# Attention's chunk loads wait for the landing of the load two chunks ahead, the first weights' load for the one ahead of it

## The chip, the cores and the metric

The kernel runs on one NeuronCore of a Trainium2 chip. The metric is the device time of one execution in microseconds (us); lower is better. TensorE (PE) multiplies matrices, VectorE (DVE), ScalarE (ACT) and GpSimd (POOL) work on elements, SyncE (SP) issues most of the DMAs, ScalarE's queue a few.

## The reference

Three layers, each on the output of the one before, all in fp32:

```python
def _attn_ref(q, k, v):            # batch 4, 8 heads, 768 steps, head_dim 64
    for t in range(S):
        state = gamma * state + einsum('bhd,bhe->bhde', k[:, :, t], v[:, :, t])
        y[:, :, t] = scale * einsum('bhd,bhde->bhe', q[:, :, t], state)

def _moe_ref(x, w_in, w_out):      # 3072 tokens, 512 -> 2048 -> 512
    h = maximum(x @ w_in, 0.0)
    return h * h @ w_out

def _moe2_ref(x, w_gate, w_val, w_out, rms_g):   # 512 -> 1536 -> 512
    xn = x / sqrt(mean(x * x) + 1e-6) * rms_g
    g = xn @ w_gate
    return silu(g) * (xn @ w_val) @ w_out
```

## The kernel before, in words

**Attention** is done in chunks of 128 steps, 24 of them (4 batches by 6 chunks, `NCH = 24`, `CH = 6`). A chunk's q, k, v and k by token lie side by side in DRAM, 1024 KB in all; a batch's last chunk needs no k by token and loads 768 KB. The chunks go into a ring of five places in SBUF, `qkv_sb[:, n % RING]` with `RING = 5`. For chunk n TensorE multiplies k by q into scores (L794), VectorE masks them (L1340); TensorE then multiplies q by the running state (L813), updates the state (L845) and multiplies v by the masked scores (L822), whose last product counts `chunk_done`. The scores of chunk n+1 are made before the rest of chunk n, so TensorE needs the load of n+1 when it begins its turn n. ScalarE scales k two chunks ahead (L973) and stores the outputs of 16 of the 24 chunks to DRAM on its own DMA queue, 256 KB each (L961); the outputs of the other eight stay in SBUF. VectorE copies the outputs out of PSUM (L1329).

**The two expert layers** follow in three tiles of 1024 tokens each. Every product is made by Strassen's scheme of seven products, and every one of these by three fp32r products of a high and a low part (L871 to L873). For this ScalarE rounds an operand to its high part and GpSimd or VectorE subtracts that from it to get the low part. A group of weights ("m") is four blocks in `raw_w`, 1024 KB; its sums and parts go to `w_ops`. The weights of the second matrices are prepared once, as 49 "items" of 512 KB that are stored to DRAM (L476) and later loaded back. The first 14 items are prepared during attention, from two sets of raw weights loaded into `raw_w` in four halves of 512 KB (L464), and some wait in places of `ops` that the first expert products need: those products start with attention's end, and ScalarE may write their operands only when the items are stored.

**The order of the loads** is written by hand in SyncE's program (L478 to L505), one queue, in this order: tables and the first three chunks in halves (L443, L446), chunks 3 and 4 (`load_chunk`, L451), then for each n from 0 to 18: wait until chunk n is done and its place is free, load chunk n+5; behind chunk 6 the first weights (`load_raw_w(0)`, L458), behind chunks 9, 11, 16 and 17 one half of the items' raw weights, behind chunk 13 the gains (2 KB). Then come the stores of the 14 items, the first two ahead of the second weights (L503), twelve behind. A load's landing is told by a semaphore of its place: `chunk_ready(n)` (L424) names the semaphore and the count for chunk n, and TensorE, ScalarE and GpSimd wait for it. GpSimd (`first_sums`, `low_w`) and ScalarE (`high_w`) work on the first weights from chunk 4 on.

Of the kernel before, what the change touches and what calls it, by code (L numbers as in the profile page):

```python
# [40 lines left out]
RING = 5  # L41
# [75 lines left out]
def updates_by(n):  # L117
    b, c = divmod(n, CH)
    return (CH - 1) * b + min(c + 1, CH - 1)
# [18 lines left out]
def build(nc, qkv, decay_rows, tables, w_f1, w_f2, w_b, rms_g, out):  # L138
# [6 lines left out]
    with ExitStack() as ctx:  # L145
# [278 lines left out]
        def chunk_ready(n):  # L424

            return loaded[n % RING], 16 * (n // RING + 1)
# [14 lines left out]
        def _(sp):  # L441
# [3 lines left out]
            def load_first_kv(n):  # L445
                sp.dma_start(qkv_sb[:, n, V:K + 1], qkv[0, n, :, V:K + 1, :]).then_inc(loaded[n], 16)  # L446

            def load_chunk(n):
                b, c = divmod(n, CH)
                kinds = 4 if c < CH - 1 else 3  # L450
                sp.dma_start(qkv_sb[:, n % RING].rearrange("p a d -> p (a d)")[:, 0:kinds * DM],  # L451
                             qkv[b, c].rearrange("p a d -> p (a d)")[:, 0:kinds * DM])\
                    .then_inc(loaded[n % RING], 16)

            def load_raw_w(m):
                src = w_f1[m % R1] if m < M1 else w_f2[(m - M1) % R2]
                dst = raw_w[:, m % 2].rearrange("p a k d -> p (a k d)")
                sp.dma_start(dst, src).then_inc(raw_w_loaded[m % 2], 16)  # L458

            def load_early_quad(quad, half):  # L460

                src = w_b[quad].rearrange("p (a d) -> p a d", a=4)[:, 2 * half:2 * half + 2, :]
                dst = raw_w[:, 1 - quad, 2 * half:2 * half + 2].rearrange("p a k d -> p a (k d)")
                sp.dma_start(dst, src).then_inc(quad_loaded[0], 16)  # L464
# [17 lines left out]
            load_first_kv(1)  # L482
            load_first_kv(2)
            for n in range(FIRST, RING):
                load_chunk(n)
            for n in range(NCH - RING):
                sp.wait_ge(chunk_done, n + 1)
                if n % CH == 0:
                    sp.wait_ge(state_done, updates_by(n))
                load_chunk(n + RING)  # L490
                if n == 1:
                    load_raw_w(0)
                if n in (4, 6):
                    load_early_quad(0, (n - 4) // 2)
                if n == 8:
                    sp.dma_start(gains[:], rms_g).then_inc(consts_loaded, 16)
                if n in (11, 12):
                    sp.wait_ge(w_lo, 7)
                    load_early_quad(1, n - 11)
# [1405 lines left out]
```

## Time and profile before

| | us |
|---|---|
| median of 3 runs | 1064.64 (1064.18 to 1065.65) |
| the profiled execution | 1066.32 |
| its span, first to last instruction | 1064.6 |
| TensorE busy | 1055.0 (99%) |
| VectorE busy | 876.7 (82%) |
| ScalarE busy | 610.1 (57%) |
| GpSimd busy | 331.8 (31%) |
| granted clock of TensorE | 1.000 |

The page of the profile gives the busy time of each engine as the union of its instructions' times. The chain that ended last is followed back from the last instruction, at each step to what released it. The list of waits tells which engine stood idle, before which of its lines, and what ended the wait; "issue" there is idle time for which the profile shows nothing that was waited for. A DMA appears twice: as an instruction on its issuing queue (SPq, ACTq) with its start, and in the list of DMA issues with its size and the time from issue to landing. The list of DMA queues counts the packets that moved in a stretch: q1 is SyncE's queue, q10 ScalarE's, q8 and q14 carry instructions. Shares of the DMA are of 16 engines.

### The profile page before, as it was taken

How to read it: one execution, taken by the hardware profiler on the slowest of the kernel's cores; microseconds unless marked ns; L12 is line 12 of the kernel's file. 1: busy time of each engine (PE TensorE's matmuls, PEld its weight loads, DVE VectorE, ACT ScalarE, POOL GpSimd, SP SyncE). 2: the span in 40 equal slices, each digit the busy share in tenths (PEclk: the TensorE clock that was granted, in tenths of full speed). 3: DMA queues.
4: the chain of work that ended last, by engine and by line, in shares of the span. 5: the costliest groups of instructions: out<-in, count | busy, mean ns of one | idle time of the engine just before them, and what ended most of it. 6: DMA issues, size and time to landing. Idle time of an engine off the chain costs nothing.

```text
span 1064.6 us, 15660 instructions
## 1 busy us (share of the span) xinstructions
PE 1055.0 (99%) x5974; PEld 885.0 (83%) x5974; DVE 876.7 (82%) x940; ACT 610.1 (57%) x887; POOL 331.8 (31%) x244
## 2 busy tenths in 40 slices
PE   8999999999999999999999999999999999999999
PEld 7878888888888888888888888888888888888898
DVE  5877989878879878789899988978886986978684
ACT  4774775557664666654674645556454555544353
POOL 1864550004540015430034554005444102544000
DMA  9999568664438644365642335632225751130455
GB/s 370 388 417 416 208 227 272 216 198 139 178 119 277 213 139 164 139 254 195 223 143 97 119 119 220 215 119 80 60 77 153 266 189 49 53 106 21 141 187 187
DMA packets 77529, 195.69 MB, mean 184 GB/s; under 512 B 23944, under 2 KB 34184, under 8 KB 70416
## 3 DMA queue, kind: packets, MB, share of 16 engines
q1 hardware_dynamic: 74992, 189.96, 50.9%
q10 hardware_dynamic: 2464, 4.74, 1.2%
q8 instruction: 48, 0.79, 0.3%
q14 instruction: 25, 0.20, 0.1%
HBM read 152.11 MB, written 42.48 MB: 183 GB/s over the span
## 4 chain that ended last, share of the span: by engine, by line
PE 97%; DMA 2%; DVE 1%; issue 0%; ACT 0%
PE Y L871 13%; PE Y L872 13%; PE Y L873 13%; PE X L871 9%; PE Z L872 9%; PE X L872 9%; PE Z L871 9%; PE Z L873 9%; PE X L873 9%; DMA qkv_sb<-qkv 2%; PE Z L822 1%; PE X L794 1%; PE Y L794 1%; PE R L845 1%; PE Z L813 1%
## 5 line engine op out<-in xcount | busy, mean ns | idle before, releaser
L715 POOL TENSOR_TENSOR w_ops<-raw_w,w_ops 128x512 fp32r<-128x512 f32 x90 | 129.4, 1438 | 500.6 <-ACT w_ops L985 500.5
L1047 ACT CAST ops<-hid 128x1024 fp32r<-128x1024 f32 x147 | 154.7, 1053 | 162.8 <-PE Z L873 55.1
L1440 DVE TENSOR_TENSOR ops<-hid,ops 128x1024 fp32r<-128x1024 f32 x147 | 180.1, 1227 | 45.4 <-ACT ops L1047 44.9
L715 POOL TENSOR_TENSOR w_ops<-sums_w,w_ops 128x512 fp32r<-128x512 f32 x120 | 166.3, 1388 | 119.3 <-ACT w_ops L985 118.8
L871 PE MATMUL Y<-ops,w_ops 128*128 128x512 f32 x360 | 140.1, 389 | 0.0
L873 PE MATMUL Y<-ops,w_ops 128*128 128x512 f32 x360 | 140.1, 389 | 0.0
L872 PE MATMUL Y<-ops,w_ops 128*128 128x512 f32 x360 | 140.1, 389 | 0.0
L1083 ACT ACTIVATE gt<-gt 128x512 f32<-128x512 f32 x72 | 45.1, 632 | 111.6 <-DVE gt L1657 38.9
L871 PE MATMUL Y<-ops 128*128 128x512 f32 (+1 forms) x288 | 104.5, 363 | 0.0
L872 PE MATMUL Y<-ops 128*128 128x512 f32 (+1 forms) x288 | 104.4, 362 | 0.0
L873 PE MATMUL Y<-ops 128*128 128x512 f32 (+1 forms) x288 | 104.4, 362 | 0.0
L985 ACT CAST w_ops<-sums_w 128x512 fp32r<-128x512 f32 x120 | 74.3, 620 | 43.4 <-PE Y L873 17.0
L871 PE MATMUL X<-ops,w_ops 128*128 128x512 f32 x240 | 93.5, 390 | 0.0
L873 PE MATMUL Z<-ops,w_ops 128*128 128x512 f32 x240 | 93.4, 389 | 0.0
L873 PE MATMUL X<-ops,w_ops 128*128 128x512 f32 x240 | 93.4, 389 | 0.0
L871 PE MATMUL Z<-ops,w_ops 128*128 128x512 f32 x240 | 93.4, 389 | 0.0
L872 PE MATMUL Z<-ops,w_ops 128*128 128x512 f32 x240 | 93.4, 389 | 0.0
L872 PE MATMUL X<-ops,w_ops 128*128 128x512 f32 x240 | 93.4, 389 | 0.0
L871 PEld LDWEIGHTS Y<-ops,w_ops 128*128 128x128 f32 x360 | 67.6, 188 | 14.4
L873 PEld LDWEIGHTS Y<-ops,w_ops 128*128 128x128 f32 x360 | 67.6, 188 | 14.1
L872 PEld LDWEIGHTS Y<-ops,w_ops 128*128 128x128 f32 x360 | 67.6, 188 | 13.8
L1355 DVE TENSOR_TENSOR ops<-raw,ops 128x1024 fp32r<-128x1024 f32 x39 | 55.3, 1422 | 27.6 <-ACT ops L1004 27.6
(180 smaller groups left out, 2317.7 us busy)
## 6 DMA issues: line engine op xcount, KB each, us to landing
ops<-item_scratch SPq DMA_DIRECT2D x147, 512.0 KB, 3.4
raw_w<-w_f SPq DMA_DIRECT2D x30, 1024.0 KB, 4.9
qkv_sb<-qkv SPq DMA_DIRECT2D x17, 1024.0 KB, 8.9
item_scratch<-hid SPq DMA_DIRECT2D x30, 512.0 KB, 3.1
y_scratch<-hid SPq DMA_DIRECT2D x12, 512.0 KB, 5.5
raw<-y_scratch SPq DMA_DIRECT2D x3, 2048.0 KB, 9.6
raw<-w_b SPq DMA_DIRECT2D x5, 1024.0 KB, 4.9
out<-hid SPq DMA_DIRECT2D x36, 128.0 KB, 5.2
```

The source lines that it names most:

```text
L715: nc.gpsimd.tensor_tensor(w_ops[:, k, 1], front_w_source(m, k), f32(w_ops[:, k, 0]), ALU.subtract).then_inc(w_lo, 1)
L794: mm = nc.tensor.matmul(scores_ps[n % 2][:, h % 2, cols], qkv_sb[rows, n % RING, KT, cols], qkv_sb[rows, n % RING, QT, cols], start=h < 2, ...
L813: nc.tensor.matmul(y_place(n, h), state[rows, c % 2, p, :], qkv_sb[rows, n % RING, QT, P * p:P * p + P], start=p < 2, stop=False, skip_gro ...
L822: mm = nc.tensor.matmul(y_place(n, h), qkv_sb[:, n % RING, V, h * D:(h + 1) * D], masked[:, c % 2, h % 2, P * p:P * p + P], start=c == 0 a ...
L871: nc.tensor.matmul(dst, left_hi, right_hi, start=start, stop=False, skip_group_check=True)
L872: nc.tensor.matmul(dst, left_hi, right_lo, start=False, stop=False, skip_group_check=True)
L873: return nc.tensor.matmul(dst, left_lo, right_hi, start=False, stop=True, skip_group_check=True)
L985: nc.scalar.copy(w_ops[:, k, 0], front_w_source(m, k)).then_inc(w_hi, 1)
L1047: nc.scalar.copy(hop_at(n)[:, 0], hid[:, 2 * g:2 * g + 2, OPERAND[k], :]).then_inc(hop_hi, 1)
L1083: nc.scalar.activation(gt[:, i % 2, :], gt[:, i % 2, :], ACT.Silu).then_inc(gate_out, 1)
L1355: nc.vector.tensor_tensor(front_lo_at(k), raw_slot(OPERAND[k]), f32(front_hi_at(k)), ALU.subtract).then_inc(front_lo, 1)
L1440: nc.vector.tensor_tensor(hop[:, 1], hid[:, 2 * g:2 * g + 2, OPERAND[k], :], f32(hop[:, 0]), ALU.subtract).then_inc(hop_lo, 1)
```

## The change

```diff
@@ -482,13 +482,16 @@
             load_first_kv(1)
             load_first_kv(2)
             for n in range(FIRST, RING):
+                sp.wait_ge(*chunk_ready(n - 2))
                 load_chunk(n)
             for n in range(NCH - RING):
                 sp.wait_ge(chunk_done, n + 1)
                 if n % CH == 0:
                     sp.wait_ge(state_done, updates_by(n))
+                sp.wait_ge(*chunk_ready(n + RING - 2))
                 load_chunk(n + RING)
                 if n == 1:
+                    sp.wait_ge(*chunk_ready(n + RING - 1))
                     load_raw_w(0)
                 if n in (4, 6):
                     load_early_quad(0, (n - 4) // 2)
```

`FIRST` is 3. Before it issues the load of chunk n, for n from 3 to 23, SyncE now also waits until chunk n-2 has landed; before the first weights, which follow the load of chunk 6, it waits until chunk 5 has landed. The halves of the items' weights, the gains, the stores and the later weights have no wait of their own. The order of SyncE's DMAs stays.

## Rows read from the trace of the kernel before

**Rows 1.** The page's chain that ended last, by engine.
```profile
PE 97%; DMA 2%; DVE 1%; issue 0%; ACT 0%
```

**Rows 2.** Stretches: window, length and PE busy (instructions), clock, DMA share, GB/s.
```profile
12.00:86.94 74.94, 69.71 (x1346) 1.00 1.01 408
86.94:1064.60 977.66, 975.01 (x4538) 1.00 0.48 165
```

**Rows 3.** PE's waits, 12 to 87 us: total us, times, longest.
```profile
PE X L794 <- DMA qkv_sb<-qkv: 1.7, 2, 1.3
PE Z L822 <- issue: 1.5, 1, 1.5
PE Y L794 <- DMA qkv_sb<-qkv: 0.5, 1, 0.5
```

**Rows 4.** PE's timeline: start, duration, line, [idle before, releaser].
```profile
25.84 0.66 PE L822 MATMUL Z<-masked,qkv_sb 128*64 128x128 f32 x8 [1.50 <-issue]
...
65.72 1.16 PE L794 MATMUL X<-qkv_sb 64*128 64x128 f32 x16 [1.27 <-DMA qkv_sb<-qkv]
...
71.71 1.16 PE L794 MATMUL X<-qkv_sb 64*128 64x128 f32 x16 [0.44 <-DMA qkv_sb<-qkv]
```

**Rows 5.** Issues of chunks 3, 4, 6, weights, chunk 20, each above its us to landing.
```profile
3.81 0.56 SPq L451 DMA_DIRECT2D qkv_sb<-qkv  x1
qkv_sb<-qkv SPq DMA_DIRECT2D x1, 1024.0 KB, 10.5
...
4.41 0.54 SPq L451 DMA_DIRECT2D qkv_sb<-qkv  x1
qkv_sb<-qkv SPq DMA_DIRECT2D x1, 1024.0 KB, 13.5
...
15.28 0.33 SPq L451 DMA_DIRECT2D qkv_sb<-qkv  x1
qkv_sb<-qkv SPq DMA_DIRECT2D x1, 1024.0 KB, 7.0
...
15.65 1.33 SPq L458 DMA_DIRECT2D raw_w<-w_f  x1
raw_w<-w_f SPq DMA_DIRECT2D x1, 1024.0 KB, 9.1
...
60.71 0.33 SPq L451 DMA_DIRECT2D qkv_sb<-qkv  x1
qkv_sb<-qkv SPq DMA_DIRECT2D x1, 1024.0 KB, 10.9
```

**Rows 6.** DMA issues, 110.4 to 115.3 us: weights loaded into idle DMA engines.
```profile
raw_w<-w_f SPq DMA_DIRECT2D x1, 1024.0 KB, 4.7
```

**Rows 7.** Chunk 9's issue; DMA totals of 17.9:24.6, then 26:30; a store and its landing.
```profile
26.52 0.33 SPq L451 DMA_DIRECT2D qkv_sb<-qkv  x1
...
DMA packets 380, 2.81 MB, mean 420 GB/s; under 512 B 36, under 2 KB 36, under 8 KB 42
...
DMA packets 188, 1.40 MB, mean 350 GB/s; under 512 B 18, under 2 KB 18, under 8 KB 18
...
27.26 0.36 ACTq L961 DMA_DIRECT2D x_scratch<-y_sb  x1
...
x_scratch<-y_sb ACTq DMA_DIRECT2D x1, 256.0 KB, 7.4
```

**Rows 8.** DMA totals of 14.3:71.6; instruction packets in 14.3:71.6, 14.3:45, 14.3:17.9 (packets, MB, share).
```profile
DMA packets 4663, 23.23 MB, mean 405 GB/s; under 512 B 637, under 2 KB 637, under 8 KB 2663
...
q8 instruction: 9, 0.15, 1.0%
...
q8 instruction: 5, 0.08, 1.1%
...
q8 instruction: 1, 0.02, 1.8%
```

**Rows 9.** DMA queues, 23.4 to 23.6 us: the instruction packet before the 25.84 us stall.
```profile
q8 instruction: 1, 0.02, 34.3%
```

## The prediction

> **What bounds the kernel.** I began with the chain that ended last [rows 1]: TensorE is 97% of it, the loads of attention's chunks are 2%. Two stretches say where the rest lies [rows 2]: from 86.94 us on, where the first expert product starts, TensorE works 975.01 of 977.66 us, so whatever attention gains or loses is handed one for one to the end, as long as nothing new stalls the products. Before it, from 12 us, it works 69.71 of 74.94. Its waits there [rows 3] are of two kinds: 1.5 us for which no semaphore is named ("issue"), and 2.2 us for chunk loads. The timeline [rows 4] puts the first before 25.84 us and the others late: the loads of chunks 18 and 20 are waited for until 65.72 and 71.71 us. From 71.71 to the first product lie 15.2 us of work that loads hardly touch.
>
> The other resource is the DMA engines, from 12 to 86.94 us busy all the time (share 1.01) [rows 2]. When a load lands follows from its issue row and the latency row beside it [rows 5]: chunk 3 at 3.81 + 10.5 = 14.3, chunk 4 at 17.9, chunk 6 at 22.3, the weights at 24.7, chunk 20 at 71.6 us. They land in the order of issue, one of 1024 KB about 2.5 us after the other (22.3, 24.7). So the loads form one line, served in turn, that never empties. Between 14.3 and 71.6 us it carries, by the program's order, 14 chunks of 1 MB, 3 of 768 KB, the weights' 1 MB, 4 halves of the items' weights of half a MB each and 8 stores of 256 KB: 21.25 MB, at 2.5 us each 53.1 of the 57.3 us. Overhead is 4.2 us.
>
> **The change, part by part.** It adds 22 waits on SyncE and no work: one for each load of chunks 3 to 23, one for the first weights. A wait met at once costs nothing that shows. These mostly bind: chunk 3 goes at 3.81 and now waits for chunk 1, which landed before half a MB (chunk 2) and 1 MB (chunk 3), so by my estimate at 14.3 - 3.7 = 10.6; chunk 6 goes at 15.28 and waits for chunk 4, 17.9; the weights go at 15.65 and wait for chunk 5, about 1.9 us behind chunk 4; chunk 20 goes at 60.71 and waits for chunk 18, which TensorE takes up as it lands, at 65.72 [rows 4, 5]. Instead of three or four loads, two are then outstanding. Since the line is full anyway, a load begun later doesn't land later for that alone. Three terms could change it.
>
> *Does the line run dry?* A 1 MB load into idle engines lands after 4.7 us [rows 6]; 2.5 are transfer, 2.2 fixed. With the gate, load n goes when n-2 has landed and n-1 still has 2.5 us to run. That covers the fixed part with 0.3 us to spare, some 0.2 when SyncE's waking is counted. Load for load I take 0. The other bound: chunk 9 goes at 26.52, when chunk 8 alone is outstanding, and in the 4 us from 26 on the engines move 350 GB/s where 420 is the rule [rows 7]: (1 - 350/420) x 4 = 0.7 us lost, once. I stay with 0, because the isolated load holds the whole latency, and the store begun at 27.26 lies in the same 4 us. At the start the line does run dry: chunk 3 goes at 10.6 with half a MB left, and lands at 10.6 + 4.7 = 15.3, not 14.3. **+1.0 us.**
>
> *Do the engines get out of step?* TensorE's own instructions come over the same engines, in packets of 16 KB: 9 from 14.3 to 71.6 us, 5 of them before 45 us [rows 8]. One falls between the landings of chunks 3 and 4, and these are 3.6 us apart, not 2.5. I read it so: the packet holds one of sixteen engines up by 1.1 us, and a load has landed when its last engine is done. Nine of them would be 9.9 us, but all overhead is 4.2; the others are absorbed, since while one engine is held the rest go on with loads queued behind, and the next packet mostly meets an engine that is ahead. The bytes show that lead: 23.23 million went through where 21.25 x 1.0486 = 22.28 million landed [rows 8], 0.95 million or 2.3 us at 405 GB/s. With the gate an engine can be ahead by only what the cover leaves, 0.2 us, or 0.8 with a store (0.6 us) between. The five early packets then cost 0.9 each, the four late ones, among stores, 0.3 each: **+5.7 us**. Bounds: 0 (a packet that finds its engine idle) to 9.9.
>
> *What comes off?* The overhead of 4.2 us: 3.5 as the old share of these packets and the 0.7 lost around 26 us, which came from TensorE's stall of 1.5 us before 25.84 (chunk 9's load waited for the chunk that it held up). **-4.2 us.**
>
> Sum at chunk 20: 1.0 + 5.7 - 4.2 = +2.5 us. Chunk 20 sets TensorE's pace (landed 71.6, begun 71.71), so the products begin **2.5 us later**. What TensorE gains if its "issue" stall shrinks (1.5 us) comes back as waiting for those landings, so I count it at nothing; without that cover it is the first rival's gain.
>
> *Behind the new waits.* On SyncE, the first weights go some 4 us later but land, in the line, a few tenths later; GpSimd and ScalarE make of them what TensorE first reads at 86.94. Behind chunk 23's load are 14 stores of items and the second weights. Their transfers begin when the line has brought chunk 23, so they move with it, and with the products that need the room they free; TensorE stands still for 2.65 us in all behind 86.94 [rows 2], so those stores are in time today. Cost nothing; what would uncover it is a line that is shifted by more than the products are. ScalarE's scaling of k and its stores wait for the same landings and move along.
>
> **Time.** The profiled execution took 1066.32 us, its span 1064.6; with the sum it becomes 1068.8. It lies 1.68 above the runs' median of 1064.64, so for the median 1067.1 us.
>
> **Rivals.**
> *Faster: TensorE's instructions come sooner.* Place: the stall before 25.84 us; its packet moved only at 23.4 to 23.6 [rows 9], with chunk 6, the weights and chunk 7 queued. Price: 1.5 us, and up to 2.2 us of landing waits more if the line gains too: 1060.9 at best, 1062.0 with about half of the latter. It decides if chunk 20 lands at least 2 us earlier. For it: other queues do stand behind the loads, as the 256 KB store of 27.26 shows, 7.4 us to land [rows 7] for 0.6 of transfer. Against: the line is full and its work the same. Chance 0.22. The Trainium skill (DMA: Bandwidth & Descriptors, "Queues, rings and completion order") has each engine go round between queues packet by packet; by that a deep load queue would delay no other queue and this rival would win nothing, 1064.6 at best. The store's 7.4 us disagrees. The skill (Runtime: NRT & Kernel Launch, "Instruction fetch mechanics") also calls the cost of crossing an instruction block mostly hidden, which the stall of 1.5 us isn't.
> *No difference.* The cover suffices and packets fall on idle engines, so the overhead stays at 4.2: 1064.6 us. For it: a few tenths to spare by the arithmetic; against: the lead of 2.3 us now. Chance 0.26. That the waits don't bind is ruled out by the landings.
> *Dry at every load.* 0.7 us as at chunk 9, for some 15 loads: 1064.6 + 10.5 = 1075.1. Chance 0.05; stores between the later loads speak against it.
> *The forecast,* +1 to +7 us, 1067.1: chance 0.47, 0.09 of it under 0.2% (2.1 us), about what a measurement of this kernel can tell from no change.
>
> Slower: 0.38 + 0.05 = 0.43. Within 0.2%: 0.26 + 0.09 + 0.02 of the first rival = 0.37. Faster: 0.20. The range goes from inside the faster case, 1061.5, to 1071.5, where most packets show in full; the forecast's own is 1065.6 to 1071.5.
>
> **What would show it.** Right: SyncE's waits name loads; chunk 3 lands at 15.3; chunk 20 at 74 us; TensorE's waits for loads rise from 2.2 to some 6 us while "issue" falls; first product at 89.4; TensorE as dense behind it as now. Wrong: chunk 20 landed by 70 us (the first rival); 420 GB/s kept from 15 to 45 us with landings 2.5 us apart (the packets cost nothing); TensorE idle for clearly more than 2.65 us behind its first product (a cost there that I put at nothing).

## The result, and the profile after

The change costs 1.1%: 1077.28 us median of 4 runs (1075.03 to 1078.17) against 1064.41 (1063.72 to 1065.65) for the kernel before, a ratio of 1.0109, 95% interval 1.0093 to 1.0124. The forecast had the sign, but its +2.5 us should have been some +12, and the range ended at 1071.5. The profiled execution took 1078.17 us, its span 1076.4; before it was 1066.32 and 1064.6, so the two profiles differ by 11.85 us and can be compared with one another.

The page's chain that ended last, by engine, of the kernel after (for [rows 1]):

```profile
PE 89%; DMA 9%; ACT 1%; DVE 1%; issue 0%; SPq 0%; POOL 0%; ACTq 0%; DVEq 0%
```

Stretches of the kernel after, with the columns of [rows 2] (window, length, busy us and instructions of PE, PEld, DVE, ACT, POOL, then PE's clock, DMA share, GB/s):

```profile
12.00:97.45 85.45, 74.19 (x1365) 63.11 (x1360) 60.03 (x99) 50.05 (x168) 42.66 (x33) 0.94 0.96 357
97.45:1076.40 978.95, 975.93 (x4538) 817.07 (x4536) 812.79 (x833) 558.09 (x716) 285.44 (x203) 1.00 0.49 165
```

The first expert product now starts at 97.45 us instead of 86.94: 10.5 of the 11.8 us are lost ahead of it. Behind it TensorE runs as before (978.95 us instead of 977.66), so the rest is small and outside attention's loads. Ahead of it the DMA engines move 357 GB/s where they moved 408, with a busy share of 0.96 instead of 1.01.

Waits of PE from 12 to 97.4 us (for [rows 3]), then those of SyncE from 0 to 97 us:

```profile
PE X L797 <- DMA qkv_sb<-qkv: 8.8, 6, 2.4
...
PE Y L797 <- DMA qkv_sb<-qkv: 2.2, 1, 2.2
```

```profile
SPq L491 <- DMA qkv_sb<-qkv: 58.4, 17, 6.1
SPq L451 <- DMA qkv_sb<-qkv: 7.5, 2, 6.6
...
SPq L458 <- DMA qkv_sb<-qkv: 1.4, 1, 1.4
```

SyncE waits for loads 20 times, as intended. TensorE's waits for chunks rise from 2.2 to 11.0 us; its stall of 1.5 us with no releaser is gone. Issues of chunks 3, 14 and 20 of the kernel after, each above its us to landing (for [rows 5]):

```profile
10.42 0.33 SPq L451 DMA_DIRECT2D qkv_sb<-qkv  x1
qkv_sb<-qkv SPq DMA_DIRECT2D x1, 1024.0 KB, 4.8
...
49.63 0.33 SPq L451 DMA_DIRECT2D qkv_sb<-qkv  x1
qkv_sb<-qkv SPq DMA_DIRECT2D x1, 1024.0 KB, 7.4
...
73.43 0.33 SPq L451 DMA_DIRECT2D qkv_sb<-qkv  x1
qkv_sb<-qkv SPq DMA_DIRECT2D x1, 1024.0 KB, 7.9
```

Chunk 3 goes at 10.42 and lands at 15.2 us, chunk 20 at 73.43 + 7.9 = 81.3: 9.7 us later than before. DMA totals of 15.3 to 81.3 us of the kernel after, and its instruction packets there (for [rows 8]):

```profile
DMA packets 4709, 23.37 MB, mean 354 GB/s; under 512 B 639, under 2 KB 639, under 8 KB 2701
...
q8 instruction: 9, 0.15, 0.8%
```

Between the same two landings nearly the same bytes (23.37 MB for 23.23) and the same number of instruction packets, nine, take 66.0 us instead of 57.3.

The last 0.8 us of the 10.5 arise behind chunk 20's landing, from TensorE's clock. From the start of chunk 20's scores to the first expert product, in the kernel before and in the kernel after:

```profile
71.71:86.94 15.23, 14.47 (x288) 12.16 (x288) 13.89 (x22) 8.93 (x29) 8.61 (x7) 1.00 1.02 412
```

```profile
81.37:97.45 16.08, 15.96 (x289) 13.53 (x289) 11.82 (x20) 9.03 (x29) 6.37 (x5) 0.89 0.99 366
```

Nearly the same products take 1.5 us longer, and 0.6 us of idle time that stood between them before is gone. A stretch of the kernel after, 1.1 us behind the end of its wait for chunk 20, and the product that follows its wait before 31.44 us:

```profile
82.46:86.10 3.64, 3.64 (x51) 3.13 (x49) 1.72 (x3) 2.76 (x11) 1.27 (x1) 0.53 0.91 318
```

```profile
31.44 2.08 PE L797 MATMUL Y<-qkv_sb 64*128 64x128 f32 x16 [2.20 <-DMA qkv_sb<-qkv]
```

After waits of 2.1 to 2.4 us the mean granted clock of some 4 us is 0.53 to 0.64 (from 82.5 to 85.8 us alone it is 0.50, the lower level of 1.2 GHz), and a chunk's scores take 2.08 us instead of 1.16 [rows 4]. From chunk 20's landing to the first product lie 16.1 us instead of 15.3. Earlier such stretches (31.4 and 58.2 us) lie ahead of loads that are late anyway, so I count them at nothing.

### The profile page after: what moved, and what is told of

It is laid out like the page before. It is cut to its first block, busy times and chain, and to the rows that moved or that the text cites. A ratio compares the mean times of both kernels' runs of the same rounds, so it can differ in the third digit from the quotient of the medians.

```text
span 1076.4 us, 15675 instructions
## 1 busy us (share of the span) xinstructions
PE 1060.6 (99%) x5974; PEld 889.2 (83%) x5974; DVE 876.9 (81%) x940; ACT 610.2 (57%) x887; POOL 330.9 (31%) x244
## 4 chain that ended last, share of the span: by engine, by line
PE 89%; DMA 9%; ACT 1%; DVE 1%; issue 0%; SPq 0%; POOL 0%; ACTq 0%; DVEq 0%
PE Y L874 13%; PE Y L875 13%; PE Y L876 13%; PE Z L875 8%; PE X L875 8%; PE Z L876 8%; PE Z L874 8%; PE X L876 8%; PE X L874 8%; DMA qkv_sb<-qkv 7%; DMA item_scratch<-ops 2%; ACT k_dec L976 0%; ACT w_ops L988 0%; DVE sums_w L1497 0%; POOL ops L760 0%
```

## The experiments

Two theories were open. **A** is the prediction's second term: an instruction packet holds one of 16 engines, and the gate takes away the lead with which the others absorbed it. **B** is its first term with a size above 0: the load is issued too late, and engines run dry before it starts. The expectations call them so, in the wording of their time; B found its final form only with the last three kernels. Ratios are against runs of the kernel before on the same chip.

**How far ahead the gate looks.** Chunk n waits for chunk n-3, or n-1, instead of n-2. The first weights' gate also looks one load further ahead in the first of these kernels and is unchanged in the second:

```diff
-                sp.wait_ge(*chunk_ready(n + RING - 2))
+                sp.wait_ge(*chunk_ready(n + RING - 3))   # three ahead; n - 3 at the start
+                sp.wait_ge(*chunk_ready(n + RING - 1))   # one ahead; n - 1 at the start
```

> The same waits, but for the load three chunks ahead (the first weights wait for the one two ahead). Theory A, the straggler: a packet of TensorE's instructions holds up one of the sixteen DMA engines, a load has landed only when that engine is done, and with two loads outstanding the other fifteen meanwhile run empty and start cold. With three outstanding they have another 2.5 us of work, about the 2.5 us by which chunk 4's engines lay apart, so nearly all of the loss goes: chunk 20 lands at 71.5 to 74 us, total 1064 to 1067 us. Theory B, the fixed latency: the 2.2 us before and behind a transfer are longer under load than the 2.5 us of cover; three outstanding give 5.0 us, so nothing is lost at all: 1064. Theory C, that any waiting of SyncE for landings costs (by the order of loads and stores, or by what is behind it on its queue): still over 5 us slower, 1070 or more.

Three ahead: 1066.69 us (10 runs), ratio 1.0006 (0.9996 to 1.0016). The loss is gone, though SyncE still waits for loads 15 times.

> The waits are for the load directly ahead, so one chunk load at a time. Each load then takes its isolated 4.7 to 4.8 us (measured 4.8 for chunks 3 and 6 in the changed kernel), and the line is empty between any two. Both A and B: from chunk 2's landing at 11.7 some 21 loads of 4.8, less 0.6 for three of 768 KB, put chunk 23 at about 111 us, where the changed kernel has it at 91.5: some 20 us slower than the changed kernel, about 1097. A also says that the packets now cost little, because they fall on idle engines: the landings are 4.8 to 5.5 apart without outliers of 7 or 8 us. B has no say on that.

One ahead: a single run, 1114.02 us beside 1065.75. Its stretch from 12 to 87 us, and the issue of chunk 4 with its us to landing:

```profile
12.00:87.00 75.00, 50.69 (x834) 42.94 (x832) 36.80 (x61) 32.46 (x110) 25.43 (x20) 0.86 0.68 234
```

```profile
16.67 0.33 SPq L451 DMA_DIRECT2D qkv_sb<-qkv  x1
qkv_sb<-qkv SPq DMA_DIRECT2D x1, 1024.0 KB, 4.8
```

Nearly every chunk load stands alone here: chunk 3 landed at 16.66, chunk 4 went at 16.67 and landed at 21.5, 4.8 us, the isolated load of [rows 6]. So the fixed part of 2.2 us, with which the prediction reckoned, is right in attention too. The time came out 17 us above what was expected: where a store lies between two loads, they mostly land 5.7 to 5.9 us apart, and chunk 13 landed 7.4 us behind chunk 12, with an instruction packet of 2.3 us in its way. A had ruled such a landing out.

**Where the loss lies.** The same gates for chunks 3 to 11 and the weights alone; for chunks 12 to 23 alone; for chunks 3 and 4 alone; for the weights alone:

```diff
+                if n + RING < 12:       # early only; chunks 3, 4 and the weights' gate stay
+                if n + RING >= 12:      # late only; the other gates are left out
                     sp.wait_ge(*chunk_ready(n + RING - 2))
```

> The waits stay for chunks 3 to 11 and for the first weights; chunks 12 to 23 go as in the kernel before. In the changed kernel chunk 11 lands at 44.5 us and not at 40.1, so 4.4 of the 9.7 us by which chunk 20 is late arise early. If losses of the line add up, since it is never idle in the kernel before (A and B): about +4.4, less up to 1 us of lead that the engines win back: 1067.5 to 1069. If the line can catch up once loads are queued again (the rival): within 1 us of 1064.5.

> The waits stay for chunks 12 to 23 only. By the same landings 5.3 us of the loss arise here, so A and B: 1069 to 1071. A, finer: the packets between 45 and 85 us (five) each cost 1 to 2 us, seen as landings with engines far behind. The rival, that stores between the loads cover the gate and only the early waits cost: within 1.5 us of 1064.5.

> Only the waits before chunks 3 and 4 (for chunks 1 and 2). The sum of the prediction had +1.0 us here (chunk 3 landing at 15.3 in place of 14.3), and the line is never idle behind it, so A and B both say +1.0 for the landings of all chunks behind; chunk 4 with a packet at 15.9 us perhaps another 1. Total 1065.5 to 1067. The rival: the lag is eaten up by the lead of the engines before chunk 17: no difference.

> Only the first weights wait, for chunk 5's landing. SyncE is held until 19.8 us and issues chunk 7 right behind, at about 20.2 in place of 18.5. Queue at that time: chunk 6 alone, 2.5 us. By A and B this costs nothing on the line (weights 24.7, chunk 7 at 27.3), and TensorE's packet of 23.4 us has one load fewer ahead of it, so its stall of 1.5 us before 25.84 should shrink or go. The line paces the end, so the total gains little: 1063.5 to 1065. The rival, that even one short queue costs 1 us or more: chunk 7 at 28.5 or later.

Early only: 1070.24 us, ratio 1.0045 (1.0030 to 1.0060). Late only: 1070.73, 1.0051 (1.0029 to 1.0073). Start only: 1067.18, 1.0014 (1.0005 to 1.0023). Weights only: 1066.51, 1.0009 (1.0000 to 1.0018). So early and late gates each cost about 5 us, the start 1.5 us of them (1.0 was forecast) and the weights' one gate about 1, though its interval reaches down to nothing. Early only and weights only came out above what was expected (1069 and 1065 at most). The prediction had most of the cost early (packets at 0.9 us each, late ones, among stores, at 0.3); there is no such difference.

The last kernel is the cleanest view of one gate: its timeline is that of before up to 19 us. Three stretches of a microsecond each of the kernel with the weights' gate alone, and chunk 6's issue and us to landing:

```profile
19.70:20.70 1.00, 1.00 (x32) 0.83 (x34) 0.97 (x2) 0.20 (x1) 0.00 (x0) 1.00 0.57 213
20.70:21.70 1.00, 1.00 (x24) 0.83 (x19) 0.67 (x2) 0.00 (x0) 0.00 (x0) 1.00 0.76 164
21.70:22.70 1.00, 1.00 (x18) 0.97 (x16) 0.69 (x1) 0.00 (x0) 0.00 (x0) 1.00 0.95 377
```

```profile
15.45 0.33 SPq L451 DMA_DIRECT2D qkv_sb<-qkv  x1
...
qkv_sb<-qkv SPq DMA_DIRECT2D x1, 1024.0 KB, 6.8
```

Chunk 6 lands at 22.2 us, yet from 19.7 to 20.7 only 57% of the engines' time is busy: most engines have moved their share of it by then (by the landing events, explained below, 12 of 16 shares have landed by 20.8), and the weights, issued at 19.76, are not there yet. The three stretches move 754 of 3 x 420 GB/s: 1.2 us are lost. The weights land 3.7 us behind chunk 6 instead of 2.5.

**Is it the held engine?** Four one-engine copies of 17 KB behind chunks 6, 10, 14 and 18, in the kernel before and in the changed one. Each held its engine for 0.73 us:

```diff
+                if n in (1, 5, 9, 13):
+                    sp.dma_start(extra_dram[n // 4], w_f2[0, 0:17, 0:256]).then_inc(extra_done[n // 4], 16)
```

> The kernel before, with four extra DMAs of 17 rows of 1 KB, DRAM to DRAM, on SyncE's queue behind chunks 6, 10, 14 and 18 (17 rows don't divide over several engines, so each should run on one engine, as a packet of instructions does; their data are not used). A dose of the suspected cost. Theory A: with three or four loads queued the other engines go on, and the four holds of some 1 to 1.5 us, all on one engine, add up to a lag of 4 to 6 us on that engine, of which the 2 to 3.7 us by which engines lie apart anyway hide most: 0 to 2.5 us slower, 1065 to 1068. Theory B (fixed latency not covered): no effect beyond a few tenths here.

> The changed kernel (waits two ahead) with the same four extra DMAs. Theory A: each hold delays one landing and with it all sixteen engines, as the packets do at chunks 4, 12, 14, 16 and 20 (1.7 to 2.4 us over the step of the kernel before): 4 times 1.5 to 2.3 = 6 to 9 us slower than the changed kernel, so 1083 to 1086. Theory B: 17 KB on a line that is short of cover anyway: under 1.5 us slower, 1077 to 1079.

Before: 1065.45 us, ratio 1.0002 (0.9990 to 1.0015). After: 1076.70, 1.0107 (1.0086 to 1.0127), no more than the 1.0109 of the changed kernel without them. So four held engines add nothing that shows. But the copies test A only in part. Their dose is smaller than a packet's 1.1 us: less the slack of 0.2 us that A grants, four of them would cost some 2 us at most, and each of the two ratios is known to 0.0015 or 0.002, some 2 us. And none of them held the engine that a landing waited for: in the changed kernel they landed at 24.7, 41.7, 56.4 and 72.4 us, each 0.9 to 1.5 us before the last share of the chunk in front (25.8, 42.8, 57.4 and 73.9). They show that holding an engine which isn't the last costs nothing.

**One gate at a time.** The kernel before with the gate at chunks 9, 14 and 20 alone:

```diff
+                if n + RING in (9, 14, 20):
+                    sp.wait_ge(*chunk_ready(n + RING - 2))
                 load_chunk(n + RING)
```

> The kernel before, with the wait for the load two ahead only in front of chunks 9, 14 and 20, far from each other. Theory B (a load must be issued 3 to 4 us before the load in front of it lands, or every engine starts it late; two ahead leaves 2.5 to 3.2 us): the landing of chunk 14 comes about 3.6 us behind chunk 13's instead of 2.6, of chunk 20 about 3.8 behind chunk 19's instead of 3.1, of chunk 9 3.6 instead of 3.4, on the first engine to finish as on the last; first product 1.5 to 2.5 us later than before, 1066.5 to 1067.5. Theory A (a load starts in time on the engines that are free, and only an engine held by an instruction packet is late): the first engine's landings keep their steps, and the time stays within 0.5 us of before unless a packet falls just there.

1069.14 us, ratio 1.0033 (1.0021 to 1.0044): 3.5 us for three gates, more than the 1.5 to 2.5 expected. Chunks 13 and 14 of the kernel with three gates, issue and us to landing:

```profile
38.99 0.33 SPq L451 DMA_DIRECT2D qkv_sb<-qkv  x1
...
qkv_sb<-qkv SPq DMA_DIRECT2D x1, 1024.0 KB, 9.4
```

```profile
46.01 0.33 SPq L451 DMA_DIRECT2D qkv_sb<-qkv  x1
...
qkv_sb<-qkv SPq DMA_DIRECT2D x1, 1024.0 KB, 4.9
```

and four stretches of it around chunk 14's issue (last two columns DMA share and GB/s):

```profile
44.90:45.90 1.00, 1.00 (x36) 0.83 (x30) 1.00 (x2) 0.27 (x1) 1.00 (x2) 1.00 0.77 288
45.90:46.90 1.00, 1.00 (x20) 0.83 (x18) 0.55 (x3) 1.00 (x5) 1.00 (x2) 1.00 0.23 90
46.90:47.90 1.00, 1.00 (x20) 0.88 (x22) 1.00 (x2) 1.00 (x6) 1.00 (x1) 1.00 0.76 180
47.90:48.90 1.00, 1.00 (x25) 0.83 (x26) 1.00 (x2) 1.00 (x5) 1.00 (x2) 1.00 0.92 377
```

Chunk 13 "has landed" at 38.99 + 9.4 = 48.4 us, and chunk 14 is issued 2.4 us ahead of that. But at 45.9 to 46.9 the engines are 23% busy, so on the mean some 12 of 16 have nothing to do: a landing is told when the last engine is done. The four stretches move 935 of 4 x 420 GB/s, 1.8 us are lost. The loss need not show in the load's own landing. Chunk 14 lands at 50.9, only 2.5 us behind chunk 13, because the slowest engine was still fed in time; the fast ones have lost their lead, and it is chunk 15 that lands 4.3 us later, with an instruction packet at 50.4 in its way. At the other two gates it does show: chunk 9 lands 6.1 us behind chunk 8 (3.0 before), chunk 20 4.2 us behind chunk 19 (3.1 before).

The trace has the landing of every engine's share of a load. The first share of chunk 9 lands 4.4 us behind the first share of chunk 8, that of chunk 14 4.6 us behind chunk 13's, and that of chunk 20 4.7 us behind chunk 19's, where the kernel before has 3.1, 2.5 and 2.7. So even the engines that were never held begin these loads late. That is what B forecast; A, by which only a held engine is late, fails here.

From the same events I worked out, for single loads, the lead on the mean engine (mean landing of the load in front minus the issue) and what the load lost (step of the mean landing minus its transfer: 2.47 us, 0.65 more where a store lies between, 0.05 for the gains):

```
kernel, load                issued  load in front: mean, last   lead   step  transfer  lost  lead+lost
one ahead, chunk 4          16.67          16.38   16.66       -0.29   4.84    2.47    2.37    2.1
after, chunk 6              20.12          20.15   21.88        0.03   4.58    2.47    2.11    2.1
three gates, chunk 14       46.01          46.45   48.41        0.44   4.21    2.52    1.69    2.1
three gates, chunk 9        27.15          28.38   29.52        1.23   4.39    2.47    1.92    3.2
weights only, weights       19.76          20.84   22.21        1.08   3.68    2.47    1.21    2.3
after, chunk 20             73.43          74.69   76.25        1.26   4.62    3.12    1.50    2.8
after, chunk 9              31.46          33.68   34.40        2.22   3.45    3.12    0.33    2.5
three gates, chunk 6        15.59          18.34   19.62        2.75   2.49    2.47    0.02    -
```

Lead and loss add up to 2.1 to 2.8 us, in one case 3.2 (chunk 9 there has one engine 2.9 us behind the mean). The sum is the time from issue to mean landing less the transfer, so it is each load's fixed part; the last row shows that nothing is lost once the lead exceeds it. A load must be issued that long before the mean engine is done with the one in front: the fixed part of 2.2 us, or somewhat more.

How much lead is left at a gate depends on how far the last engine of the landing trails the mean, and there instruction packets come in. In the kernel that looks one ahead, chunk loads that stand alone and met no packet in mid-transfer have a last engine 0.2 to 0.5 us behind the mean; loads that met one (at 31.5, 45.9, 59.2 and 64.7 us) have it 1.3 to 2.0 us behind. In full lines such a lag stays for several loads: 1.4 us from chunk 4 to chunk 8 in the kernel before. And the loss follows the lag. The gate of chunk 6 opens with chunk 4's last engine, and chunk 5, of 768 KB, gives less cover than others. With chunk 4's last engine 2.0 us behind its mean (changed kernel) chunk 6 lost 2.1 us; with it 1.1 us behind (early only, and the changed kernel with copies) 1.2 and 1.5 us. So A was wrong on who is late and right on one part of the cause: packets make most of the lag for which the gate holds every engine back.

**More lead.** Each chunk's load as two DMAs with a semaphore each (consumers wait for both). The control waits for the whole chunk two ahead; the other kernel waits, from chunk 5 on, for its first half:

```diff
+                for lo, hi, done in ((0, 2, qk_loaded), (2, kinds, loaded)):
...
-                sp.wait_ge(*chunk_ready(n + RING - 2))
+                sp.wait_ge(*qk_half(n + RING - 2))
```

> The changed kernel with each chunk's load from chunk 3 on issued as two DMAs (q and k by head, then v and k by token), consumers and gates waiting for both: the same gates, the same lead of 2.5 us. Control for the next kernel. Both theories: as the changed kernel, 1076 to 1079.

> As the control with two DMAs for each chunk, but the gate from chunk 5 on waits for the first half of the chunk two ahead, so a load goes some 1.25 us sooner (lead about 3.7 us instead of 2.5). Theory B: the lead now suffices at most loads; the time falls from the control's about 1077 to 1067 to 1070, landings of the first engine again 2.5 us apart. Theory A (stragglers only): engines may be ahead by 1.4 us instead of 0.2, so packets of 1.1 us are mostly absorbed too, but landings of the first engine were never late; the same 1067 to 1070, told apart by the first engine's steps. If the lead is not what matters (the time lies in what else the gate moves, or in TensorE's clock), 1075 or more.

Control: 1079.82 us, ratio 1.0135 (1.0121 to 1.0149), a little above the 1076 to 1079 expected; splitting may cost something by itself, though the interval just meets that of the changed kernel. With the earlier gate: 1072.22, 1.0058 (1.0042 to 1.0073). The only difference is that loads are issued about 1.25 us sooner, and it is worth 7.6 us. The expected 1067 to 1070 is missed by 2 us; the gates at the start, unchanged here, cost 1.5 us alone and may be most of that, which no run separates. The stretch from 12 to 87 us of the control, of the kernel with the earlier gate, and of the one that looks three ahead:

```profile
12.00:87.00 75.00, 61.15 (x1120) 51.64 (x1120) 50.70 (x83) 43.73 (x149) 37.10 (x29) 0.95 0.96 338
```

```profile
12.00:87.00 75.00, 63.39 (x1196) 53.92 (x1198) 53.41 (x88) 47.55 (x161) 39.35 (x31) 0.98 0.98 364
```

```profile
12.00:87.00 75.00, 71.20 (x1355) 60.65 (x1356) 59.09 (x100) 49.69 (x168) 44.55 (x33) 1.00 1.02 413
```

338, 364 and 413 GB/s: the throughput follows the lead.

**Every second gate.** In the changed kernel, by the landing events, the lead on the mean engine alternates: 1.25, 1.28, 1.26 and 1.12 us at chunks 14, 16, 20 and 22, but 2.95, 4.06, 3.57 and 2.99 at 15, 17, 19 and 21. A late chunk n lengthens the time in which chunk n+1, issued when n-1 landed, is already queued; then n+2 is short again. If so, gates at the even chunks alone should cost what all of them do:

```diff
+                if n + RING in range(12, NCH, 2):
+                    sp.wait_ge(*chunk_ready(n + RING - 2))
```

> The kernel before, with the wait for the load two ahead only in front of chunks 12, 14, 16, 18, 20 and 22, half of the gates of the kernel with the gates from chunk 12 on (+5.6 us by its mean ratio). Theory B in its present form: the gate opens when the slowest engine has landed chunk n-2; the mean engine is then 1.3 us further and has 1.2 us of chunk n-1 left, and a load needs some 2.5 us from its issue to be moving, so 1.3 us are lost. The load behind it is not short of lead (chunk n-1 landed 2.5 us or more before n could), so in the changed kernel only every second gate costs anything. Then these six gates alone cost as much as all twelve: 1070 to 1072, chunks 14, 16, 18, 20, 22 landing 3.7 to 5 us behind the one before on the mean of the engines. If each gate has its own price, half of it: 1067.5 to 1068.5. If only engines held by instruction packets count, 1066 to 1068.

1071.07 us (8 runs), ratio 1.0054 (1.0035 to 1.0073). Six gates cost as much as the twelve of the late-only kernel (1.0051), and half of that, 1.0025, is outside the interval. Of the single landings, chunks 16, 20 and 22 came 4.3, 3.9 and 4.5 us behind the one in front on the mean, as expected; chunks 14 and 18 only 3.0 and 3.1 (behind the gains and a half of the items' weights, which lie directly in front of them). That half gives 18 its lead. At 14 the arithmetic of the table holds: chunk 12's last engine was only 0.6 us behind its mean, where the changed kernel has 2.1, so the gate opened early enough to leave 2.1 us of lead, and 0.5 us were lost. The profiled execution, 1068.92 us, is the shortest of the eight.

## Why the prediction was right or wrong

**What bounds the kernel: right.** What attention loses is handed on one for one: 10.5 us at the first product, 11.85 in the time.

**The start: right.** Chunk 3 at 15.2 us (15.3 forecast); the gates there alone cost 1.5 us for 1.0.

**"Load for load I take 0": this is the step that failed.** "With the gate, load n goes when n-2 has landed and n-1 still has 2.5 us to run." The fixed part of 2.2 us, which that was to cover, is right. The 2.5 us are not: they run from the last engine of n-2 to the last of n-1, but the gate opens with the last engine while most engines are already well into n-1. On the mean engine 1.0 to 1.3 us are mostly left where the gate costs (0.03 at chunk 6), so 1.2 to 2.1 us are lost each time, at about every second load. The number was within reach: the prediction's next paragraph has a lead of 2.3 us of most engines on the last, and the sum never subtracted such a lag from the cover. With the 1.4 us by which the last engine of chunks 4 to 8 trails the mean in the kernel before, 2.5 - 1.4 = 1.1 us are left against 2.2. Its own other bound, 0.7 us a load and 1075.1 in all ("Dry at every load", chance 0.05), came nearest, with a price too small and a count too large. What spoke against that rival, the stores between the later loads, doesn't hold: late gates cost 5.4 us, early ones 4.8.

The Trainium skill (DMA: Bandwidth & Descriptors, "Why a DMA increments its semaphore by 16 and not by 1") says that a DMA's engines finish independently and only the full count means that all has landed. The traces here agree: with three gates, chunk 13's first share landed at 45.8 us and its last at 48.4, and in between, from 45.9 to 46.9, the engines were 23% busy. They add what it means for a gate.

**"Do the engines get out of step?" +5.7 us: the right ingredient in the wrong sum.** It saw that a packet holds one engine and that the gate spares no room for that. But it charged every packet once, at 0.9 us or 0.3, against 0.2 us of slack. The runs show a price per gate: six gates cost what twelve do, late gates as much as early ones, and what counts is how far the last engine trails when the gate opens, whether its packet is new or old. Chunk 20 tells that all engines are late, not the held one: its last engine is 2.5 us behind the mean before (71.66 and 69.12) and 2.0 after (81.33 and 79.31), while the mean itself comes 10.2 us later. That nine packets at the term's upper bound, 1.1 us each, would give 9.9 us, near the measured loss, is chance as far as these runs tell. How much would be lost without any packet isn't shown: no run had none.

**"What comes off", -4.2 us: wrong.** TensorE's stall of 1.5 us did go, as in the kernel with the weights' gate alone. But as far as the totals tell, little of the overhead in the line came off; the new loss lies on top. So the first rival's mechanism is real and brings nothing here. Its evidence, a store that took 7.4 us to land because it stood behind the loads, is weak: from 25 to 80 us these stores take 7.9 us (median) in the kernel before, 7.3 with two loads outstanding and still 6.2 with one.

**Behind the new waits, 0: nearly right.** TensorE stands 3.02 us behind its first product instead of 2.65; with 0.9 us more of busy time that is 1.3 us that the forecast put at nothing. The clock, +0.8 us net ahead of the first product, it had not at all.

**Sum.** Forecast +1.0 + 5.7 - 4.2 = +2.5 at chunk 20; measured +9.7: 1.0 for the start and 8.7 for a lead that is too short. That the sign came out right is partly luck: it rested on +5.7 against -4.2, and neither showed as it was reckoned. Not one of the kernels with gates beat the kernel before.

## What to carry to other kernels

Before a load is made to wait for another's landing, work out its lead on the mean engine: what is queued behind that landing, less the time by which the landing's last engine trails the others (mostly 1.1 to 2.1 us at the gates here), must exceed the fixed part of a lone load (2.2 us here). With 1 MB loads that meant three outstanding, not two. A transfer that looks hidden because "the line is full" is hidden only while the line is full on every engine.

## What the runs showed of the hardware

- The 16 engines of one queue drift apart: a chunk's last engine came up to 2.5 us behind their mean in the kernel before. For lone loads it was 0.2 to 0.5 us, and 1.3 to 2.0 us when an instruction packet (16 KB, about 1 us on one engine) fell into the transfer.
- A load into engines that have run dry started about 1 us after its issue, and its first packets of 8 KB mostly took 0.4 to 1.4 us instead of 0.31 (single packets in the trace of the kernel that looks one ahead, chunks 4 and 6).
- A load that starts late need not show in its own landing, but can in the next: chunk 14 2.5 us behind chunk 13, chunk 15 4.3 behind chunk 14.
- Waits of TensorE of 2.1 to 2.4 us were followed by some 4 us at a granted clock of 0.53 to 0.64; waits of 1.5 us in the kernel before and of 1.85 us in the changed one (before 73.41 us) left it at 1.00.
